# Strassen's seven block products for the first layer of the dense experts

## The reference

```python
# 1. attention with a threshold: 4 x 8 heads, 576 x 64, out -> x (2304, 512)
scores = where(q @ k.T * scale >= max - tau, ..., -1e9); attn = softmax(scores); x = attn @ v
# 2. sparse experts: each token through one of 8 experts (512 -> 1024 -> 512)
e = argmax(x @ w_gate); x = gate * (relu(x @ w1[e]) @ w2[e])
# 3. dense experts: every token through all of 4 experts
N, D, E, F = 2304, 512, 4, 1024
p = domain_probs / (domain_probs.sum(-1, keepdims=True) + 1e-09)
for e in range(E):
    h = np.maximum(x @ w1[e], 0.0)
    out += p[:, e:e + 1] * (h @ w2[e])
```

## Time and profile before

| | before |
|---|---|
| median of three runs | 1445.99 us (1445.89 to 1447.39) |
| the profiled execution's own time | 1443.94 us |
| its span, first to last instruction | 1442.2 us |
| mean granted TensorE clock in it | 0.999 of full |
| PE, DVE, ACT, POOL busy | 99, 50, 40, 11% |
| dense stage, first to last matmul | 639.57 to 1438.46 us |

### The profile page before, as it was taken

One profiled execution on the slowest core, in us unless ns is written; L12 is line 12 of the kernel. 1 busy time (PEld: TensorE's weight loads), 2 busy tenths in 40 slices (PEclk: granted clock), 3 DMA queues, 4 the chain that ended last, 5 costly groups with the idle time before them and its releaser, 6 DMA issues.

```text
span 1442.2 us, 27631 instructions
## 1 busy us (share of the span) xinstructions
PE 1422.2 (99%) x10501; PEld 1252.6 (87%) x10501; DVE 718.5 (50%) x1111; ACT 575.5 (40%) x1030; POOL 160.7 (11%) x328
## 2 busy tenths in 40 slices
PE   8999999998999999999999999999999999999999
PEld 6777777777888888899999999999999999999998
DVE  7888888856777777763222252222332222522221
ACT  6777777755666666642122231111221111311111
POOL 3222222212112222220000000000000000000000
PEclk9999999999999999999999999999999999999999
DMA  4322222107888889872000030000110000100001
GB/s 92 69 67 64 67 67 67 36 19 227 279 287 281 279 294 298 290 223 84 1 0 1 0 117 1 1 0 1 60 59 0 1 0 1 60 22 23 22 23 44
DMA packets 156076, 127.28 MB, mean 88 GB/s; under 512 B 88768, under 2 KB 129824, under 8 KB 156000
## 3 DMA queue, kind: packets, MB, share of 16 engines
q1 hardware_dynamic: 148160, 103.94, 24.3%
q0 software_dynamic: 6640, 21.97, 4.4%
q10 hardware_dynamic: 1200, 0.26, 0.1%
HBM read 110.02 MB, written 16.12 MB: 87 GB/s over the span
## 4 chain that ended last, share of the span: by engine, by line
PE 91%; DVE 3%; DMA 3%; ACT 2%; issue 2%; SPq 0%; POOL 0%; DVEq 0%; ACTq 0%; POOLq 0%
PE front L939 9%; PE front L938 9%; PE front L937 9%; PE back L686 6%; PE back L924 6%; PE back L926 6%; PE back L925 6%; PE front L924 5%; PE front L926 5%; PE front L925 5%; PE front L711 4%; PE back L938 3%; PE back L939 3%; PE back L937 3%; PE front L724 2%; DMA ring<-in_moe_w 2%
## 5 line engine op out<-in xcount | busy, mean ns | idle before, releaser
L1131 ACT ACTIVATE hth<-front 128x384 fp32r<-128x384 f32 (+1 forms) x132 | 60.9, 462 | 503.3 <-PE front L926 502.8
L937 PE MATMUL front<-wh,hth 128*128 128x512 f32 x584 | 229.2, 392 | 0.0
L939 PE MATMUL front<-wh,htl 128*128 128x512 f32 x584 | 227.7, 390 | 0.0
L938 PE MATMUL front<-wl,hth 128*128 128x512 f32 x584 | 227.5, 390 | 0.0
L1442 DVE TENSOR_TENSOR wl<-ring,wh 128x1024 fp32r<-128x1024 f32 x160 | 192.1, 1223 | 57.8 <-ACT wh L1122 55.3
L1122 ACT CAST wh<-ring 128x1024 fp32r<-128x1024 f32 x160 | 164.7, 1053 | 60.6 <-DMA ring<-in_moe_w 60.2
L924 PE MATMUL front<-xch,wh 128*128 128x384 f32 (+1 forms) x528 | 169.4, 321 | 1.1 <-DVE htl L1456 0.7
L924 PE MATMUL back<-xch,wh 128*128 128x384 f32 (+1 forms) x528 | 169.2, 320 | 0.8 <-DVE htl L1456 0.7
L926 PE MATMUL front<-xch,wl 128*128 128x384 f32 (+1 forms) x528 | 169.3, 321 | 0.0
L925 PE MATMUL front<-xcl,wh 128*128 128x384 f32 (+1 forms) x528 | 169.2, 320 | 0.0
L925 PE MATMUL back<-xcl,wh 128*128 128x384 f32 (+1 forms) x528 | 169.0, 320 | 0.0
(11 more groups left out here) (247 smaller groups left out, 2491.6 us busy)
## 6 DMA issues: line engine op xcount, KB each, us to landing
ring<-in_moe_w SPq DMA_DIRECT2D x160, 512.0 KB
tokens_x<-x_nat SPq DMA_DIRECT2D x16, 288.0 KB, 4.4
x_nat<-compact_y POOLq DMA_DIRECT2D x6, 768.0 KB, 6.5
raw<-in_q SPq DMA_DIRECT2D x32, 128.0 KB, 2.5
vv<-in_v SPq DMA_DIRECT2D x32, 128.0 KB, 2.2
raw<-in_k SPq DMA_DIRECT2D x30, 128.0 KB, 2.6
vv<-in_v SPq DMA_DIRECT2D x64, 16.0 KB, 2.1
out<-x_nat SPq DMA_DIRECT2D x3, 256.0 KB, 2.1
```

Source lines behind the costliest of these rows:

```text
L937: pe.matmul(acc_bank[t], hth[:, f, ts], w2_block(wh, f), start=f == 0, stop=False)
L938: pe.matmul(acc_bank[t], hth[:, f, ts], w2_block(wl, f), start=False, stop=False)
L939: last = pe.matmul(acc_bank[t], htl[:, f, ts], w2_block(wh, f), start=False, stop=f == KF - 1)
L1131: act.activation(hth[:, f, 0:n], hb(f, n), ACT.Relu).then_inc(s_hh, 1)
```

## The change

**Block products.** For 768 tokens the product x @ w1[e] is seen as two by two blocks: D in halves of 256, features in halves of 512, tokens in halves of 384. The eight block products become seven (Strassen's scheme in Winograd's form). The factors are four quarters of w1 and three more sums of them (S1 to S4, one in the place of A21), and likewise for x (T1 to T4). POOL forms the sums of weights (`mixes`), DVE those of tokens (`x_mixes`), before they are rounded and split, so each side has seven blocks to split in place of four. A block product for 128 features is six matmuls of 384 columns.

**Combining.** P1 is copied to one (ACT), P6 + P1 gives two, P7 is accumulated on P6 in PSUM and gives three, P2 is accumulated on P1, P3 on P5, P4 on P6 and P7; DVE adds in one, two and three (`sum_2`, `sum_3`, `sum_22`, `sum_21`, `sum_12`). Then relu and split as before (`rest`).

**Order.** The outer loop is over three groups of 768 tokens, the inner over four experts. The sums of outputs lie in rows, six tiles, written out after each group; before, x_nat held all 18. The second layer runs in two halves of three tiles (`down_half`). The next expert's quarters of w1 are loaded into w1r, which shares its memory with w1l, once the products that read a quarter are done, and w2 likewise into dn_r. All six token tiles of a group are turned in one place, the first six within the last sparse slot.

The core of the diff, in the order SP, POOL, PE (`product` to `expert`), DVE (from `x_mixes(0)`, behind the last sparse slot):

```diff
+            def up_part(e, slot, i, j, done):
+
+                sp.dma_start(w1r[:, slot, :, :],
+                             w1[e][2 * j * P:2 * (j + 1) * P, i * (FF // 2):(i + 1) * (FF // 2)].rearrange("(k p) f -> p k f", p=P)).then_inc(done, 16)
...
+            up_part(0, A21, 1, 0, s_a21)
+            up_part(0, A22, 1, 1, s_a22)
+            up_part(0, A11, 0, 0, s_a11)
+            up_part(0, A12, 0, 1, s_a12)
             chosen(LAST, 1)
-            with sp.Fori(0, E2) as e:
-                pieces(e + NS, w1[e], w2[e])
...
+            def fetch(q, e):
+
+                wait(sp, s_p1, 4 * q)
+                up_part(e, A11, 0, 0, s_a11)
+                wait(sp, s_p2, 4 * q)
+                up_part(e, A12, 0, 1, s_a12)
+                wait(sp, s_p7, 4 * q)
+                up_part(e, A21, 1, 0, s_a21)
+                wait(sp, s_p4, 4 * q)
+                up_part(e, A22, 1, 1, s_a22)
+                wait(sp, s_o, 6 * q)
+                down_parts(e)
...
+            def mixes(q):
...
+                pool.tensor_tensor(w[S1], w[A21], w[A22], ALU.add).then_inc(s_mixed, 1)
...
+                pool.tensor_tensor(w[S2], w[S1], w[A11], ALU.subtract).then_inc(s_mixed, 1)
+                pool.tensor_tensor(w[S3], w[A11], w[A21], ALU.subtract).then_inc(s_mixed, 1)
...
+                pool.tensor_tensor(w[S4], w[A12], w[S2], ALU.subtract).then_inc(s_mixed, 1)
...
+            def product(to, s, w, x, start):
+
+                fs = slice(s * P, (s + 1) * P)
+                for kk in range(2):
+                    pe.matmul(to[:, 0:CH], w1h[:, w, kk, fs], x2h[:, x, kk, :], start=start and kk == 0, stop=False, skip_group_check=not start)
+                    pe.matmul(to[:, 0:CH], w1h[:, w, kk, fs], x2l[:, x, kk, :], start=False, stop=False, skip_group_check=not start)
+                    last = pe.matmul(to[:, 0:CH], w1l[:, w, kk, fs], x2h[:, x, kk, :], start=False, stop=kk == 1, skip_group_check=not start)
+                return last
...
+            def p7(q, p, s):
+
+                ready(q, p, s, S3)
+                pe.wait_ge(s_u2, 4 * q + s + 1)
+                product(bank_b[s % 2], s, S3, T3, False).then_inc(s_p7, 1)
...
+            def expert(p, e):
...
+                p1(q, p, 0)
+                p6(q, p, 0)
+                p1(q, p, 1)
+                p2(q, p, 0)
+                p7(q, p, 0)
+                p5(q, p, 0)
+                for s in range(1, 4):
...
+                    p6(q, p, s)
+                    p4(q, p, s - 1)
+                    p3(q, p, s - 1)
+                    p2(q, p, s)
+                    p7(q, p, s)
+                    p5(q, p, s)
+                    if s < 3:
+                        p1(q, p, s + 1)
+                down_half(q, 0, 0, 1)
+                p4(q, p, 3)
+                p3(q, p, 3)
+                down_half(q, 0, 1, 4)
...
+                down_half(q, 0, 4, KF)
...
+                down_half(q, 1, 0, KF)
...
+            x_mixes(0)
+            for i in range(3):
+                x_rest(0, i)
+            for i in range(3, 7):
+                x_rest(0, i)
+                w_rest(0, i)
             y_out(LAST, 1)
...
+            def expert(p, e):
...
+                for s in range(1, 4):
+                    sum_2(q, s)
+                    sum_21(q, s - 1)
+                    sum_12(q, s - 1)
+                    rest_21(q, s - 1)
+                    rest_12(q, s - 1)
+                    rest_11(q, s)
+                    sum_3(q, s)
+                    sum_22(q, s)
+                    rest_22(q, s)
+                    if s == 2:
+                        w2_rest(q, 0, 0)
+                    elif s == 3:
+                        w2_rest(q, 1, 2)
+                sum_21(q, 3)
+                sum_12(q, 3)
+                rest_21(q, 3)
+                rest_12(q, 3)
+                w2_rest(q, 2, 1)
+                w2_rest(q, 3, 3)
...
+                if q < E2 * NW - 1:
+                    for i in range(7):
+                        w_rest(q + 1, i)
+                add_up(p, e, 0)
```

More of the change, by code:

```diff
@@ L71 @@
 TF = NT - CH // P
+WIDE = 2 * CH
+NW = TOK // WIDE
+WT = WIDE // P
+STAGE = 4
+HB = KF * NS
+A11, S2, A12, S3, S1, A22, S4 = range(7)
+B11, T2, B21, T3, T1, T4, B22 = range(7)
+A21, B12 = S3, T3
 NCST = 10
@@ L350, in build @@
         s_dn, s_y = sem("s_dn"), sem("s_y")
-        s_ld = [sem(f"s_ld{c}") for c in range(NC)]
+        s_rows, s_more = ([sem(f"s_{n}{p}") for p in range(NW)] for n in ("rows", "more"))
         s_tab, s_oi = sem("s_tab"), sem("s_oi")
@@ L971, in slot @@
                 if final(m, b):
[L972 removed]
+                    first_rows()
                 else:
@@ L978, in slot @@
                     pe.wait_ge(s_y, tiles_to(m, b))
-                down(j, j, n, s_dn, pair=b == 0 and not final(m, b))
+                down(j, j, n, s_dn, pair=b == 0 and not final(m, b), closing=final(m, b))
             turn_x(0, 0)
@@ L1010, in _ @@
+            for p in range(NW):
+                expert(p, 0)
+                with pe.Fori(1, E2 - 1) as e:
+                    expert(p, e)
+                expert(p, E2 - 1)
         @block.scalar
@@ L1562 @@
+            for p in range(NW):
+                for e in range(E2):
+                    expert(p, e)
+            add_up(NW - 1, E2 - 1, 1)
 _INS = ["q", "k", "v", "tau", "moe_w_gate", "moe_w1", "moe_w2", "moe2_domain_probs", "moe2_w1", "moe2_w2"]
```

520 lines of the change are left out of this document (392 added, 128 removed).

## The result

| | before | changed kernel |
|---|---|---|
| median | 1446.16 us (1445.89 to 1447.39) | 1405.1 us (1404.95 to 1407.36) |
| profiled execution | 1443.94, span 1442.2 | 1407.36, span 1405.6 |
| first turning of dense tokens, to the last matmul | 627.35 to 1438.46: 811.1 | 630.13 to 1401.93: 771.8 |
| matmuls of 384 columns, dense first layer | 2304 | 2016 |

What follows compares the result with a forecast made beforehand. The prediction took the dense stage to last as long as its PE matmuls, other engines having room. -50.0 + 5.4 + 1.7 + 1.1 = -41.8 us from 1445.99 gave 1404.2; own range 1399 to 1411, stated range 1399 to 1421.

Steps and rivals of the forecast that it cites:

- What goes: 50.0 us: Dense first layer: 288 matmuls of 384 columns go, each worth its issue interval of 0.1736 us, 50.0 us saved.
- Nothing inside an expert: Within an expert's feature blocks and weight preparation, every hand-off is done before PE needs it, so no wait is added.
- u: The prediction's clock within an expert: time since PE began that expert's last feature block.
- rival A: Dense stage: POOL and DVE stretch each other, PE waits 9 to 29 us in all, 1412 to 1432; chance 18%.
- POOL and DVE: 1.1 us: POOL's sums beside DVE's second-layer weight remainders: 0.1 us for each of 11 experts, bounds 0 and 19 us.
- Border: 5.4 us: Sparse to dense: PE waits 5.4 us at expert 0's first p7 for DVE's first sum; bounds 3 and 8.
- Clock: 1.7 us: Behind the border's wait the granted clock may fall, losing 1.7 us of work; bounds 0 and 2.5.
- Loads at the last sparse slot: covered: Dense weight loads issued first delay the last slot's by up to 7 us; covered, if not up to 3 us.
- The sum: Whole kernel: saved matmuls, border wait, clock and POOL beside DVE total -41.8 us, giving 1404.2.
- B: Feature-block loop doesn't close: PE waits up to 1 us in each of 36 blocks, 1420 to 1440; chance 5%.
- C: Next expert's single weight buffer: POOL sums above 4.8 us make PE wait; slower than before from 5.8 us; chance 4%.
- D: Border is covered after all, at full clock: 1396 to 1399; chance 6%.

Runs made afterwards that it cites:

- e2_eight: Changed kernel with product S1 x T1 computed twice in every feature block, bringing 288 matmuls back: 1452.68 us.
- e1_same: The changed kernel run once more, unaltered, as base for the others: 1403.62 us, dense part 771.82.
- e5_turn: Changed kernel with the first-half additions ahead of the last three weight remainders in DVE's list in the two turning experts: 1402.16 us.
- e7_pool_copy: Changed kernel with each of POOL's four sums replaced by a copy of one operand, so products use other weights: 1400.48 us.
- e4_border: Changed kernel with the border reordered: two weight blocks ahead of the token tiles, last sparse outputs after the first feature block's sums: 1397.01 us.
- e6_pool_double: Changed kernel with each of POOL's four sums per expert computed twice: 1484.63 us.
- e9_outputs_later: Changed kernel with only the last sparse slot's two outputs moved behind the first feature block's sums in DVE's list: 1401.51 us.

## Why the prediction was right, step by step

**What goes: 50.0 us.** Right. Its 2016 matmuls follow at 0.173 to 0.174 us, one pass of a plain expert is 61.9 us (61.8 predicted), and the eighth product, taken in again, adds 24 x 0.173 us to each (e2_eight). One argument for it was not sound: a line through two intervals (174 and 227 ns) leaves the same rest for both whatever a change of banks costs. The products' own interval shows that the conclusion holds.

**Nothing inside an expert.** Right for PE: no wait but one of 0.5 us for `three`, in one execution, and the new sums take 0.55 to 0.56 us. Right for the wrong reason at one edge. The sums of POOL took 2.4 to 3.2 us, not 1.8, and end at u = 24.3, not 19.6. The slack of 11 us at the next p1 took that. The narrow place, the last remainder of the second layer's weights, shows as the doubled row 4.56 (against 2.36 alone, 2 x 1.22 less overlap), and PE did not feel it. That was luck: the sums started at u = 13.7, not 12.4, so the first of the two remainders was nearly done when they began, and the pair ended at u = 17.4 (e1_same), where PE needs it at 18.5. From 12.4 on, my own chain with 2.4 us a sum gives POOL to 14.8, DVE to 16.0, POOL to 18.4, DVE to 19.6 (an estimate): 1.1 us late in each of 11 experts, 12 us in all, as in rival A.

**POOL and DVE: 1.1 us.** The mechanism of rival A is real, and the price was 2.5 (e5_turn). In my forecast it cost 0.1 us in each of 11 experts; it costs nothing in nine and 1.2 us in each of the two turning ones, where I had written "DVE ends near 39, PE wants them at 43.5". DVE's list took 2.2 us longer at the second layer's remainders and 4.8 at the token sums, 7 in all. That step failed, in size and in place; A had it in place, but asked for 9 us at least. The sum survived since the error is small.

A POOL addition and a DVE operation with two SBUF inputs take turns here: 3.03 and 3.05 us for token sums of 0.96, beside POOL's of 3.1. This is what the Trainium skill, page "SBUF — State Buffer", section "SBUF: two separate sides", states as an exclusive lock for a whole instruction, and the trace agrees: a DVE operation of 1.22 us ends 1.1 us after the POOL instruction that was there before it, whether that is a sum or a copy, and one of 0.96 ends 0.8 after it. The Trainium skill's page "GPSIMD Engine Reference", section 3.1, gives 4497 ns for an addition of 2048 columns, half of which, as an estimate, is 2.25; measured are 2.40 alone. That page was nearer than my line through POOL's short rows.

**Border: 5.4 us.** Right place, right releaser, 4.0 us at p7 and 0.6 for `one` just ahead of it. PE reached p7 at 648.9 in this execution, 5.1 behind p1, and the list ended at 652.8; both are later than in the prediction's times, since the sparse stage ended later. Measured from the first turning, PE wanted p7 at 18.8 us where I had 17.6, and the sum was done at 22.7 as against 23.0.

**Clock: 1.7 us.** Right sign, and as near as one number can be. Behind the same wait of 4.0 us the matmuls at half pace cost 2.0 us in the profiled execution, 2.8 in e1_same and 1.6 in e7_pool_copy; filling the wait gave 2.75 back against e1_same.

**Loads at the last sparse slot: covered.** Right. No wait for a load there, and the late sparse stage of the profiled execution was chance (e1_same).

**The sum.** Predicted -50.0 + 5.4 + 1.7 + 1.1 = -41.8. Measured in the dense part, from e1_same: -50.0 + 7.9 (border and clock, e4_border) + 2.5 (turning, e5_turn) = -39.6, against differences of 39.3 to 39.8. The losses are 10.4 in place of 8.2. The first profiled execution comes to the same 771.8 by chance: its clock cost 0.7 us less, and its wait for `three` 0.7 more. The medians' 41.1 agrees with the forecast as closely as it does partly by chance too, since the sparse stage moves it by up to 3 us.

**Rivals.** B: no waits in the blocks. C: its mechanism exists and sets in when it is provoked (e6_pool_double). Its arithmetic gives 4 x (5.4 - 4.8) = 2.4 us per expert for a doubled sum of 5.4, and 3.2 to 3.5 were measured. D: not here, but e4_border makes it so, 1397.0, inside its 1396 to 1399.

## What to carry to other kernels

Where PE is busy at full clock and waits for nobody, a removed matmul is worth its issue interval, and the work that replaces it costs nothing as long as each hand-off is walked with its slack. What remains is at the joints, where one engine's list for the new stage stands ahead of the first item that PE needs: order it by what PE wants first and fill the engine's earlier idle time. A wait of PE of 3 to 4 us can be worth up to twice its length, because the clock falls behind it: 4.6 us of waits cost 7.9 (e4_border), and with waits of 3.2 to 3.5 a pass grew by 4.8 to 6.3 us (e6_pool_double). Waits of 1.0 us cost no clock here. Before work is put on GpSimd, look at what VectorE does in the same microseconds: operations of both that have all their operands in SBUF took turns here instead of overlapping, down to a copy of six columns.

## What the runs showed of the hardware that I had not expected

- GpSimd: 2.40 us for an addition of two 1024-column float32 operands in SBUF, undisturbed, and 1.05 us for a copy. A line through additions of 25 and 192 columns gave 1.8.
- VectorE's operation with two SBUF inputs starts its work when the GpSimd instruction that was there first ends, and so ends its own length less 0.1 us after it: 0.96 becomes 3.0, 2 x 1.2 becomes 4.56. A copy of 6 columns with one input in SBUF goes from 0.18 to 2.0; a subtraction with an input in PSUM stays at 0.68. Taking turns lengthens GpSimd's too, 2.4 to 3.2.
- Behind one and the same wait of 4.0 us the clock cost between 1.6 us (e7_pool_copy) and 2.8 (e1_same), as the stretch at half clock was shorter or longer and more or less of it fell into the wait. Filling the wait with useless matmuls gave 2.75 back; behind a wait of 2.6 us it cost 1.6 (e9_outputs_later), behind one of 1.0 nothing.
